# Four reorderings across stages, and the first batch's value differences replaced by a third product

## The reference, cut to what matters

```python
# stage 1: 8 heads of 64, a window of 128 keys, a bias linear in the distance
mask = (rel >= 0) & (rel < window)
scores = np.where(mask, scale * q @ k.T + bias, -1e9)
attn = softmax(scores)          # sum + 1e-9 in the denominator
x = attn @ v
# stage 2: gated unit with a product over positions
h = relu(x @ w_in); u, v = h[..., :512], h[..., 512:]
v_n = (v - mean(v)) / sqrt(var(v) + 1e-6)
gated = u * (w_spatial @ v_n + b_spatial)
y = gated @ w_out
# stage 3: 4 experts, each a causal attention of width 64; the 2 best per token by y @ w_gate
for e in range(E):
    a = softmax(causal(scale * (y @ wq[e]) @ (y @ wk[e]).T))
    out += weight_of_expert(e) * (a @ (y @ wv[e]) @ wo[e])
```

## Time and profile before

| | |
|---|---|
| median of 3 runs | 496.9 us (496.26 to 498.81) |
| the profiled execution's own time | 496.05 us |
| its span in the profile | 494.2 us |
| PE busy | 474.0 us (96%) |
| DVE busy | 320.9 us (65%) |
| ACT busy | 271.7 us (55%) |
| POOL busy | 213.6 us (43%) |

### The profile page before, as it was taken

How to read it: one execution, slowest core, us unless ns; L and a number is a source line. 1 busy time by engine, 2 the same in 40 slices (tenths; PEclk the granted TensorE clock), 3 DMA queues, 4 the chain that set the end, 5 groups by cost and what they waited for, 6 DMA issues and landing times.

```text
span 494.2 us, 10632 instructions
## 1 busy us (share of the span) xinstructions
PE 474.0 (96%) x3794; PEld 404.1 (82%) x3794; DVE 320.9 (65%) x1247; ACT 271.7 (55%) x822; POOL 213.6 (43%) x378
## 2 busy tenths in 40 slices
PE   8689989999999999999999999999999999999996
PEld 5457989899776789999776779999876779999874
DVE  6886875257778855437778865436777975335783
ACT  5667563246676744235666654335666663335663
POOL 4494628222344526742253525760443442461431
PEclk9999999999999999999999999999999999999999
DMA  7927520003201073002311063001311000000111
GB/s 235 320 55 217 201 86 0 1 2 76 91 22 44 2 197 91 1 1 48 109 34 44 1 184 106 0 2 40 95 44 56 1 1 2 0 2 8 42 43 54
DMA packets 33512, 31.64 MB, mean 64 GB/s; under 512 B 6002, under 2 KB 24434, under 8 KB 33460
## 3 DMA queue, kind: packets, MB, share of 16 engines
q1 hardware_dynamic: 33460, 30.97, 20.6%
HBM read 23.88 MB, written 4.72 MB: 58 GB/s over the span
## 4 chain that ended last, share of the span: by engine, by line
PE 73%; DVE 14%; ACT 7%; issue 3%; POOL 2%; DVEq 0%; POOLq 0%
PE bank L1385 16%; PE bank L1387 15%; PE bank L1386 15%; PE bank L1372 6%; PE bank L1450 6%; ACT p L825 4%; PE bank L1412 3%; DVE ring L936 3%; PE bank L1614 3%; PE bank L1629 2%; PE bank L1651 2%; DVE p L1170 2%; PE bank L1391 2%; PE bank L1392 1%; POOL ring L542 1%
## 5 line engine op out<-in xcount | busy, mean ns | idle before, releaser
L542 POOL TENSOR_SCALAR ring<-ring,r 128x128 f32<-128x128 f32 x144 | 62.4, 447 | 80.1 <-DVE r L956 79.8
L628 POOL TENSOR_SCALAR p<-p,r,wgt 128x128 f32<-128x128 f32 (+3 forms) x64 | 38.6, 616 | 92.9 <-DVE wgt_last L1217 49.9
L656 ACT ACTIVATE ring<-ring,neg 128x128 f32<-128x128 f32 x144 | 56.7, 396 | 23.9 <-DVE ring L947 19.4
L825 ACT ACTIVATE p<-p,neg 128x128 f32<-128x128 f32 (+4 forms) x72 | 41.7, 580 | 31.9 <-DVE neg L1170 31.9
L936 DVE CUSTOM_DVE_ANT_0 ring<-bank,bias 128x256 f32<-128x256 f32 (+1 forms) x128 | 43.7, 385 | 6.1 <-PE bank L1372 5.6
L1372 PE MATMUL bank<-k,q 64*128 64x256 f32 (+2 forms) x320 | 39.0, 372 | 2.8 <-DVE neg L936 2.8
L592 POOL TENSOR_TENSOR g_lo<-uT,g_hi 128x288 fp32r<-128x288 f32 x32 | 26.8, 862 | 32.1 <-ACT g_hi L791 32.1
L1385 PE MATMUL bank<-g_hi,w_c_hi 128*128 128x288 f32 x128 | 38.3, 299 | 2.1 <-DVE k_lo L1273 2.1
L1385 PE MATMUL bank<-w_spatial_hi,vn_hi 128*128 128x288 f32 x128 | 37.9, 296 | 2.3 <-DVE uT L1149 2.3
L1385 PE MATMUL bank<-x_hi,w_in_hi 128*128 128x288 f32 x128 | 38.2, 298 | 0.0
L1387 PE MATMUL bank<-x_hi,w_in_lo 128*128 128x288 f32 x128 | 37.7, 294 | 0.0
(11 more groups left out here) (193 smaller groups left out, 1447.7 us busy)
## 6 DMA issues: line engine op xcount, KB each, us to landing
v_in<-v SPq DMA_DIRECT2D x16, 256.0 KB, 3.9
out<-o_sb SPq DMA_DIRECT2D x16, 256.0 KB, 2.0
q<-qT SPq DMA_DIRECT2D x15, 256.0 KB, 4.5
k<-kT SPq DMA_DIRECT2D x15, 256.0 KB, 4.8
v_minus_v_of_tile_above<-v SPq DMA_DIRECT2D x9, 256.0 KB, 3.9
w_in_raw<-w_in SPq DMA_DIRECT2D x4, 512.0 KB, 5.7
w_cat_raw<-wcat SPq DMA_DIRECT2D x1, 1544.0 KB, 7.1
w_spatial_raw<-wsT SPq DMA_DIRECT2D x1, 1152.0 KB, 8.6
```

What stands on the lines that cost most here:

```text
L542: last = nc.gpsimd.tensor_scalar(p, p, r1[:, i % 2, h:h + 1], 0.0, ALU.mult, ALU.add)
L628: nc.gpsimd.tensor_scalar(p, p, r3[:, i % 2, e:e + 1], by, ALU.mult, ALU.mult).then_inc(s3_sd, 1)
L656: nc.scalar.activation(x, x, ACT.Exp, bias=neg1[:, u % SLOTS1:u % SLOTS1 + 1], scale=-1.0, accum_out=sum1[:, i % 2, h:h + 1]).then_inc(s1_ ...
L825: nc.scalar.activation(p, p, ACT.Exp, bias=neg3[:, w % 4:w % 4 + 1], scale=-1.0, accum_out=sum3[:, i % 2, es[0]:es[0] + 1]).then_inc(s3_ex, 1)
```

## The change

Seven edits. (1) In batch 0 the product with the values has three terms instead of two: the whole block times v of the tile above, the masked block times v of the tile itself, and the masked block times the negated v of the tile above. ACT makes the negated tiles (`negate_v`, at m = 1, 3, 5, 7) in the place of `v_step`; POOL makes no difference in batch 0. (2) The masks of stage 3 are zeroed by ACT at the start, not by POOL at m = 3. (3) The zero rows of the last tile go to `v_in`. (4) On DVE the pieces of `wcat_lo` stand with those of `woT_lo` among the gates 4 to 7, not ahead of all gates. (5) On ACT `high_qk(4)` stands ahead of `exp3(0)`, in all batches. (6) On ACT `high_z(0)` stands between `exp3(8)` and `exp3(9)`, in all batches. (7) The counts of the semaphore of the differences start at batch 1.

```diff
--- before.py
+++ after.py
@@ -267,11 +267,13 @@
         s_qk_in = [sem(f"qk_tile_{t}_in") for t in range(NT)]
         s_v_in = [sem(f"v_tile_{t}_in") for t in range(NT)]
         s_vz0 = sem("v_step_zero_rows")
+        s_mz = sem("causal_masks_zero")
         s_warm = sem("warm_operand_zero")
         s_pair_in = [sem("first_tile_of_pairs_0_and_1_in"), sem("first_tile_of_pairs_2_and_3_in")]
         s1_sc, s1_bi, s1_ex = sem("s1_scored"), sem("s1_biased"), sem("s1_exped")
         s1_t, s1_h, s1_pv = sem("s1_transposed"), sem("s1_pt_copied"), sem("s1_pv_done")
         s1_h2 = sem("s1_pt_second_copied")
+        s_vneg = sem("v_negated")
         s_diag, s_vd, s1_cb = sem("diagonal_mask_ready"), sem("v_steps"), sem("s1_blocks_joined")
         s1_dn, s1_rc, s1_sd = sem("s1_denominator"), sem("s1_reciprocal"), sem("s1_scaled")
         s1_xh, s1_xl = sem("s1_xt_hi"), sem("s1_xt_lo")
@@ -499,7 +501,7 @@
 
                     link(nc.gpsimd.affine_select(out=causal[:], in_=causal[:], compare_op=ALU.is_ge, fill=MASKED, base=0,
                                                  pattern=[[-1, P]], channel_multiplier=1))
-                    link(nc.gpsimd.memset(masks[:], 0.0))
+                    pool.wait_ge(s_mz, 1)
                     link(nc.gpsimd.tensor_copy(masks[:, 512 + LAST + 512 - P:512 + LAST + 512], causal[:]))
                     for odd in range(2):
                         link(nc.gpsimd.tensor_copy(masks[D * odd:D * odd + D, 512:512 + LAST], causal[0:LAST, 0:LAST]))
@@ -518,12 +520,6 @@
             nc.gpsimd.affine_select(out=diag[:], in_=diag[:], compare_op=ALU.is_ge, fill=0.0, base=0,
                                     pattern=[[1, P]], channel_multiplier=-1).then_inc(s_diag, 1)
 
-            def first_v_step(t):
-                pool.wait_ge(s_v_in[t - 1], 16)
-                pool.wait_ge(s_v_in[t], 16)
-                r = rows(t)
-                nc.gpsimd.tensor_tensor(v_step[0:r, t - 1], v_in[0:r, t], v_in[0:r, t - 1], ALU.subtract).then_inc(s_vd, 1)
-
             def v_steps(b):
 
                 pool.wait_ge(s_vs_in, 16 * NT * b)
@@ -531,7 +527,7 @@
                     r, at = rows(t), v_step[0:rows(t), t - 1]
                     above = v_step[0:r, t - 2] if t > 1 else v_first[0:r]
                     nc.gpsimd.tensor_tensor(at, at, above, ALU.subtract).then_inc(s_vd, 1)
-                    pool.wait_ge(s_vd, (NT - 1) * b + n + 1)
+                    pool.wait_ge(s_vd, (NT - 1) * (b - 1) + n + 1)
 
             def scale1(b, g):
 
@@ -567,8 +563,6 @@
                     for g in (2 * m + 3, 2 * m + 4):
                         if g < NG1:
                             scale1(b, g)
-                        if first and g < NG1 and g % 4 == 1:
-                            first_v_step(g // 4)
                     if first and m in TABLES_AT:
                         tables(TABLES_AT.index(m), 2 * m + 5)
                 pool.wait_ge(s1_xl, NT * (b + 1))
@@ -657,8 +651,10 @@
                                          accum_out=sum1[:, i % 2, h:h + 1]).then_inc(s1_ex, 1)
 
             act.wait_ge(s_warm, 1)
-            nc.scalar.copy(v_step[LAST:P, NT - 2], pt_hi[LAST:P, 0, 0:D].bitcast(F32).unsqueeze(1).to_broadcast([P - LAST, H, D])
+            nc.scalar.copy(v_in[LAST:P, NT - 1], pt_hi[LAST:P, 0, 0:D].bitcast(F32).unsqueeze(1).to_broadcast([P - LAST, H, D])
                            ).then_inc(s_vz0, 1)
+            nc.scalar.copy(masks[:].rearrange("p (a c) -> p a c", c=LAST),
+                           pt_hi[:, 0, 0:LAST].bitcast(F32).unsqueeze(1).to_broadcast([P, 1024 // LAST + 1, LAST])).then_inc(s_mz, 1)
             exp1(0, 0)
             exp1(0, 1)
             exp1(0, 2)
@@ -701,6 +697,10 @@
                 def high_x(i):
                     act.wait_ge(s1_pv, NG1 * b + END1[i] + 1)
                     nc.scalar.copy(x_hi[:, :, tok(ORDER1[i])], xt_of(i)).then_inc(s1_xh, 1)
+
+                def negate_v(t):
+                    act.wait_ge(s_v_in[t], 16)
+                    nc.scalar.activation(v_step[:, t], v_in[:, t], ACT.Copy, scale=-1.0).then_inc(s_vneg, 1)
 
                 def relu_v(i):
                     act.wait_ge(s1_vm, NT * b + i + 1)
@@ -751,6 +751,8 @@
                             exp1(b, 2 * m + 4)
                     if m == ND1 - 3:
                         exp1(b, NG1 - 1)
+                    if first and m % 2 and m < ND1 - 1:
+                        negate_v(m // 2)
                     for half, at in W_IN_AT.items():
                         for k in range(KT):
                             if first and at[k] == m:
@@ -873,9 +875,9 @@
                 copy_v3(1)
                 copy_v3(NT - 1)
                 exp_logits(0)
+                high_qk(4)
                 exp3(0)
                 exp3(1)
-                high_qk(4)
                 exp3(2)
                 exp3(3)
                 high_qk(5)
@@ -888,7 +890,7 @@
                 copy_v3(2)
                 copy_v3(3)
                 for m in range(ND3):
-                    for i in range(NT - 2):
+                    for i in range(1, NT - 2):
                         if m == DEND3[i] + 1:
                             high_z(i)
                     for i in (NT - 2, NT - 1):
@@ -899,6 +901,8 @@
                         if m == DEND3[i] + 2:
                             copy_out(b, i)
                     for w in units3(m):
+                        if w == 2 * E + 1:
+                            high_z(0)
                         exp3(w)
                     if more and m >= ND3 - 3:
                         exp1(b + 1, m - (ND3 - 3))
@@ -1128,20 +1132,18 @@
                 if not first:
                     dve.wait_ge(s2_um, 8 * (b + 1))
                     nc.vector.memset(v3[LAST:P, AT3[NT - 1]], 0.0).then_inc(s_vz3, 1)
-                if first:
-                    for d in range(KT):
-                        dve.wait_ge(s_fsh, d + 1)
-                        nc.vector.tensor_tensor(wcat_lo[:, d, 0:CUT], wcat_raw[:, d, 0:CUT], wcat_qk_hi[:, d, :].bitcast(F32),
-                                                ALU.subtract).then_inc(s_fsl, 1)
-                    for d in range(KT):
-                        dve.wait_ge(s_fsh, KT + d + 1)
-                        nc.vector.tensor_tensor(wcat_lo[:, d, CUT:CW], wcat_raw[:, d, CUT:CW], wcat_v_hi[:, d, :].bitcast(F32),
-                                                ALU.subtract).then_inc(s_fsl, 1)
+                def low_w_cat(d, c0, c1, high, n):
+                    dve.wait_ge(s_fsh, n)
+                    nc.vector.tensor_tensor(wcat_lo[:, d, c0:c1], wcat_raw[:, d, c0:c1], high[:, d, :].bitcast(F32), ALU.subtract
+                                            ).then_inc(s_fsl, 1)
+
                 for i in range(8):
                     a, dt = divmod(i, 4)
                     c = slice(HALF * a, HALF * a + HALF)
                     if first and i >= 4:
                         d = i - 4
+                        low_w_cat(d, 0, CUT, wcat_qk_hi, d + 1)
+                        low_w_cat(d, CUT, CW, wcat_v_hi, KT + d + 1)
                         dve.wait_ge(s_fsh, 2 * KT + d + 1)
                         nc.vector.tensor_tensor(woT_lo[:, d, :], woT_raw[:, d, :], woT_hi[:, d, :].bitcast(F32),
                                                 ALU.subtract).then_inc(s_fsl, 1)
@@ -1438,7 +1440,11 @@
                     if m % 2 == 0:
                         pe.wait_ge(s_v_in[max(qb - 1, 0)], 16 * (b + 1))
                         if qb:
-                            pe.wait_ge(s_vd, (NT - 1) * b + (qb if first else NT - 1))
+                            if first:
+                                pe.wait_ge(s_v_in[qb], 16)
+                                pe.wait_ge(s_vneg, qb)
+                            else:
+                                pe.wait_ge(s_vd, (NT - 1) * b)
                         if first and qb == NT - 1:
                             pe.wait_ge(s_vz0, 1)
                         if i >= 2:
@@ -1462,6 +1468,8 @@
                         product(g, v_in[:, qb - 1], 0, True, False)
                         if g % 2 == 0:
                             pe.wait_ge(s1_h2, ND1 * b + m + 1)
+                        if first:
+                            product(g, v_in[:, qb], 1, False, False)
                         product(g, v_step[:, qb - 1], 1, False, True)
 
                 def v_product(i, k):
```

## The result

| | before | after |
|---|---|---|
| median of 14 runs each | 496.93 us (495.23 to 498.81) | 498.53 us (497.52 to 499.85) |
| ratio, 95% interval | | 1.0036 [1.0022, 1.0049] |
| the profiled execution's own time | 496.05 | 497.78 |
| its span | 494.2 | 496.1 |
| PE, DVE, ACT, POOL busy | 474.0, 320.9, 271.7, 213.6 | 476.5, 321.3, 274.2, 206.3 |

The change costs 1.6 us, 0.36%. The 1.6 is small only because large terms of both signs meet in it.

A forecast was written before the change was run, and what follows sets the result against it. TensorE was taken to bound the kernel, so savings count only where it waits. Terms +0.3 + 2.4 + 1.4 - 1.5 = +2.6 us on the profiled 496.05 gave 498.65, predicted as a 499.5 median; range 495.3 to 503.0.

The forecast's parts named there:

- D: Stage 3, four batches: high_z(0) ahead of exp3(9) on ACT removes PE's wait before the first output product, -1.5 us.
- the turns: Before the fold, batch 0: DVE and POOL alternate at SBUF, one whole instruction each; fold starts 2.4 us later.
- part A: Stage 1, batch 0: third value product and masks zeroed on ACT; added matmuls against POOL's relief, net +0.3 us.
- The fourth rival: Stage 1, batch 0: all of PE's idle time is gained, -0.7 us there, time 498.5; chance 0.08.
- Part B: Stage 2, batch 0: wcat_lo among gates 4 to 7; PE's gate wait goes, but the fold starts late, +2.4 us.
- The first rival: Before the fold: DVE slips its instructions between POOL's, fold not late, -1.5 us there, time 495.6; chance 0.22.
- second rival: Fold, batch 0: PE's idling lowers the clock for 3 to 7 us, costing 1.5 to 3.5, near 502; chance 0.20.
- Part C: Stage 3, four batches: high_qk(4) ahead of exp3(0) on ACT; low_qk(4) still stands behind reciprocal3(0), 0.36 each, +1.4 us.

The follow-up runs named there:

- `g_lo` held back: Changed kernel, but POOL starts its first g_lo only when DVE has made all twelve low parts; 492.89 us against 496.57 before, 0.9928.
- part B alone: Kernel before with only the wcat_lo pieces moved among the gates 4 to 7; 500.15 us against 496.89, 1.0068.
- the DVE order freed: Changed kernel with low_qk(4) ahead of reciprocal3(0) on DVE; 496.14 us against 496.57 before, 1.0004.
- The best kernel: Changed kernel, g_lo held for the low parts, low_qk(4) ahead of reciprocal3(0), batch 0 values with two products and POOL's differences; 490.28 us against 497.06, 0.9864.
- the kernel with the 18 matmuls: Changed kernel with 18 matmuls of 512 columns ahead of the fold, into a bank the fold overwrites; 496.53 us against 496.57 before, 1.0003.

## Why the prediction was right, and where it wasn't

**The time.** 499.5 was forecast and 498.53 came, within the range; for the profiled execution 498.65 and 497.78. Part of that agreement is luck. In the trace the clock cost 1.67, for which the sum had no term; against it stand D, 0.8 better than its term, the turns and part A, each 0.4 better, and a start-up that was 0.6 earlier by chance. The fourth rival names the same time (498.5), but for another reason, a gain of 0.7 in stage 1, and that gain didn't come.

**Part A**, forecast +0.3, measured -0.07 at the end of part 0 and -0.2 in the medians (interval -0.6 to +0.8): right within what can be told. Its steps held: the transposes came at 31.55 where 31.7 was estimated, and behind them the extra matmuls count. What the step left unsaid is how unlike its pieces are: zeroing the masks on ACT gives 1.07 by itself, and the third product in place of the differences costs 1.0.

**Part B**, the place and the mechanism were right: PE goes on behind part 0 with no wait, reaches the fold at 79.03 (79.7 forecast), waits 4.35 us (4.8) and starts at 83.38 (84.5), 0.67 of these differences being the earlier start of the whole stage. The turns cost +2.0 where +2.4 stood. The first rival, no turns, is refuted by `g_lo` held back: undisturbed the fold starts at 80.07, near the 80.5 worked out for that case. What failed is the weight of the **second rival**, the clock, at 0.20. It came in each trace in which PE waited over 4 us before the fold: the changed kernel (eight matmuls, 1.6 us), part B alone (eleven, 2.2) and the DVE order freed (twelve, 2.4), all inside the 1.5 to 3.5 given. All 32 executions of these three kernels have a mean clock of 0.992 to 0.997. The forecast took the absence of a fall behind 2.28 us of waiting as evidence that there would be none behind 4.8. It was none: one row shows that a wait of that length can pass, not that a longer one does. And the profiled execution was an exception among its own, as 52 of 60 others of the kernel before have a mean clock of 0.997 or less.

**Part C**, forecast 0.36 a batch, measured 0.31 in each: right, by its own steps. DVE's reciprocal step started 0.29 ahead of `low_qk(4)` where 0.3 was taken. Freeing DVE takes the wait away, which shows the reason.

**Part D**, forecast -1.5, measured -2.3 in the trace and -3.0 alone in the medians. The mechanism was right, the term was mis-sized. It added up the idle time of the rows, 1.33, and 0.2 for the end. But a matmul that doesn't wait starts before the record of the one ahead ends: the first output product now starts 0.16 us after the matmul ahead of it, whose record is 0.33 long. What a wait costs is the distance of the starts less what it would be without the wait, here 0.58 to 0.60 a batch where the rows say 0.31 to 0.40. The same reading error, the other way round, hides the two small waits of 0.22 in the kernel with DVE's order freed.

**Left open:** why the clock falls behind a wait of about 2.3 us in one execution and not in the next, and whether the falls that the mean clocks tell of all lie there: one of seven traces with that wait has one. Also open is how much of the spread of the kernel before (495.2 to 498.8) they make. The best kernel, with no wait over 1.5 us, spread by 0.06 us in four runs, but one of those four has a mean clock of 0.997 and the same time, so a fall can also lie where it costs nothing. And the kernel with the 18 matmuls spread from 496.1 to 497.4 over eight executions at 1.000, so there are other causes of spread.

## What to carry to other kernels

When an instruction is moved earlier or later on one engine, ask what the engine next to it does in the new place: the same order of the twelve low parts gained 1.35 us or cost about 3, by whether POOL worked in SBUF beside them. When a copy is moved on one engine, move its reader on the other too, or the reader's queue keeps it where it was. Price a wait of TensorE by the starts of its matmuls, not by the idle time shown, and where a wait is added ahead of a dense stretch, count the clock with it: here 1.6 to 2.4 us on top of 2.0. And look at the clock of many executions before taking one profile's 1.00 for the rule.

## What the runs showed of the hardware that was not expected

- The clock can fall after PE has resumed. Behind a wait of 2.29 us PE first ran on at 2.4 GHz for 1.6 us and only then, for some 14 matmuls, at 1.2 GHz (a 288-column matmul every 0.24 us instead of 0.13), in one of seven traces. Behind 4.35 us it ran on at 2.4 GHz for 0.8 us before the fall; behind 4.41 and 4.29 us in two other traces the clock was down before PE resumed, and PE ran its first matmuls at 1.2 GHz.
- Two engines that alternate in SBUF wait for each other's instruction: a 260-column subtraction took 1.04 us beside POOL and 0.42 alone, one of 512 columns up to 1.30 instead of 0.68, and POOL's own 1.05 instead of 0.78.
- The start-up differs from run to run: the same five warm-up matmuls took 2.24 and 1.42 us (one every 0.43 us, or one every 0.23), and what came next was 0.59 us earlier. Over the four traces whose program is the same up to there, the transposes behind them start between 8.57 and 10.10. That is as large as the effect that was to be measured here, and it is in every single-profile comparison of two kernels.
